# An attention stage ahead of two feed-forward blocks: squares summed by contiguous adds, the last score chunks split in halves, row sums divided out after the weight product, and six banks for that product

## The chip, the cores and the metric

The kernel runs on one core of one Trainium2 chip. The metric is the device time of one execution in microseconds; lower is better. The engines are named as in the profile: PE (TensorE), DVE (VectorE), ACT (ScalarE), POOL (GpSimd) and SP (SyncE, which issues the DMAs here).

## The reference

There are three parts in a row. The attention is over channels: q, k and v are 6016 x 256, and the attention matrix is only 256 x 256.

```
qn = q / (norm(q, axis=rows) + 1e-6)        # one norm per channel
kn = k / (norm(k, axis=rows) + 1e-6)
s  = kn.T @ qn / tau                        # 256 x 256, summed over the 6016 rows
a  = exp(s - max(s, -1));  a /= sum(a, -1) + 1e-9
x  = v @ a                                  # 6016 x 256
h  = x @ w_in1  (256 x 2048);  x = (h - tanh(h)) @ w_out1
h  = x @ w_in2  (256 x 2048);  out = where(h > 0, h, exp(min(h, 0)) - 1) @ w_out2
```

All data is float32. In the two blocks and in v's product, each float32 operand is split into a rounded high part and a low part (`_hi`, `_lo`), and three matmul passes replace one exact product.

## The kernel before

The kernel never forms x = v @ a. It multiplies the small matrices first: wf = a @ w_in1 (256 x 2048), and block 1 then computes v @ wf. So the work falls into an attention stage that ends in wf, and a main part of 12 tiles of 512 tokens (the last one shorter) in which PE runs four groups per step in a written order (A: v @ wf, B: w_out1, C: w_in2, D: w_out2). The change touches only the attention stage. Every engine has one instruction queue, written out by hand in program order; semaphores join them, and nothing is reordered at run time.

The 6016 rows are laid out as 47 rows per partition. They are loaded in chunks (`CHUNKS`, 1, 2, 2, 2 and then ten of 4 rows) into a ring of six buffers for k and six for q. For every chunk:

- SP issues the load of k and of q (L276). From the seventh chunk on it first waits until PE has multiplied the chunk that held the buffer (`chunk_multiplied`) and ACT has squared it (`squared`). After the chunks SP issues w_in1, the first tile of v (eight DMAs, L268), w_out1; after the scores w_in2; then the second tile of v; after the weight product w_out2.
- PE multiplies each row's k (as stationary operand, in two halves m = 0, 1 of 128 channels) with q, and adds all of it up in two banks, `scores_ps` (L352; the trace calls the banks `x_ps`). One such float32 matmul shows as two instructions in the trace.
- ACT squares k and q into `k_sq` and `q_sq` (L527), and may do so only when DVE has summed the chunk before (`summed`).
- DVE sums the squares over the rows with a reduction (L671). It reads the chunk's rows and the running sum, five rows of 256 for a full chunk, with the row as the innermost index, so at a stride of 256 elements, and writes one row of 256.

Then comes the end of the stage, in which little runs in parallel. When the last sum is there, PE adds it over the partitions by matmuls with a column of ones (L371), does the half m = 0 of the last chunk and one matmul of the other half of the last but one. ACT takes the root (L549), DVE corrects it by one Newton step, inverts, and puts 1/norm of q on a diagonal (L706 to L713); PE spreads that over the partitions with a matmul by ones (L385); ACT copies it to SBUF (L558). Meanwhile PE does the remaining halves m = 1. For m = 0 and then m = 1, DVE scales the scores (L719), takes the negated row maximum (L722), ACT forms exp and the row sum (L554), DVE adds 1e-9, inverts, and scales the row (L724 to L728), PE transposes it (L360), and ACT (m = 0) or DVE (m = 1) copies the result to `aT`. Last, PE forms wf in eight products of 128 x 512 (L403, four instructions each), in the order `WF_ORDER`, into four banks; ACT rounds each to wf_hi (L532) and DVE takes the difference wf_lo (L657). A product that takes a bank again waits for the split of the product before it in that bank. Between them DVE transposes the first tile of v (L687), and both engines split four pieces of w_out1.

The main part's first groups wait for the splits of the wf columns that they read.

Of the kernel before, what the change touches and what calls it, by code (L numbers as in the profile page):

```python
# [29 lines left out]
F32 = mybir.dt.float32  # L30
# [20 lines left out]
CHUNKS = [1, 2, 2, 2] + [4] * 10  # L51
# [3 lines left out]
SUM_ROW = CH + 1 if len(CHUNKS) % 2 else 0  # L55
assert sum(CHUNKS) == ROWS

# [22 lines left out]
WF_ORDER = [(0, 0), (1, 0), (0, 1), (1, 1), (2, 0), (2, 1), (3, 0), (3, 1)]  # L80
# [7 lines left out]
def attention_ffn_kernel(nc, q, k, v, tau, w_in1, w_out1, w_in2, w_out2, out):  # L88
    ctx = ExitStack()
    with ctx:  # L90
# [26 lines left out]
        row_sum = sb("row_sum", [P, CC])  # L117

        with ExitStack() as early:  # L120
            k_ring = [sb(f"k_ring{i}", [P, CH, C], stack=early) for i in range(RING)]
            q_ring = [sb(f"q_ring{i}", [P, CH, C], stack=early) for i in range(RING)]

            k_sq, q_sq = sb("k_sq", [P, CH + 2, C], stack=early), sb("q_sq", [P, CH + 2, C], stack=early)
            prob = sb("prob", [P, CC, C], stack=early)

            rq_diag, rq = sb("rq_diag", [P, CC, P], stack=early), sb("rq", [P, C], stack=early)
# [5 lines left out]
        with ExitStack() as early:  # L133
            stage_b = sb("stage_b", [P, CC * F], stack=early)
        x2_hi, x2_lo = sb("x2_hi", [P, CC, TILE], F32R), sb("x2_lo", [P, CC, TILE], F32R)
# [12 lines left out]
        scores_ps, aT_ps, wf_ps = x2_ps, h2_ps, (h2_ps, out_ps)  # L148
# [16 lines left out]
        sum_guarded, prob_ready, prob_transposed = sem("sum_guarded"), sem("prob_ready"), sem("prob_transposed")  # L165
# [175 lines left out]
        def _(pe):  # L341
# [15 lines left out]
            def transpose_prob(m):  # L357
                pe.wait_ge(prob_ready, m + 1)
                for d in range(CC):
                    last = nc.tensor.transpose(aT_ps[m][:, d * P:(d + 1) * P], prob[:, m, d * P:(d + 1) * P], ident[:, :])  # L360
                last.then_inc(prob_transposed, 1)

            for i in range(len(CHUNKS)):
                pe.wait_ge(loaded_k[i % RING], 16 * (i // RING + 1))
                pe.wait_ge(loaded_q[i % RING], 16 * (i // RING + 1))
                if i == len(CHUNKS) - 1:

                    pe.wait_ge(ones_ready, 1)
                    pe.wait_ge(summed, 2 * len(CHUNKS))
                    for col, (sq, m) in enumerate(((q_sq, 0), (q_sq, 1), (k_sq, 0), (k_sq, 1))):  # L370
                        last = nc.tensor.matmul(norms_ps[:, col:col + 1], sq[:, SUM_ROW, m * P:(m + 1) * P], ones[:, 0:1],  # L371
# [3 lines left out]
                if i < len(CHUNKS) - 2:  # L375
# [5 lines left out]
            scores(i - 1, 1, range(1))  # L381
            pe.wait_ge(rq_on_diagonal, CC)
            for m in range(CC):

                last = nc.tensor.matmul(rq_ps[:, m * P:(m + 1) * P], ones[:, :], rq_diag[:, m, :], start=m == 0, stop=True,  # L385
                                        skip_group_check=True)
            last.then_inc(rq_spread, 1)
# [9 lines left out]
            for n, (g, m) in enumerate(WF_ORDER):  # L397
                if g < 2:
                    pe.wait_ge(aT_ready[m], 1)
                else:  # L400
                    pe.wait_ge(wf_split, WF_ORDER.index((g - 2, m)) + 1)
                for d in range(CC):
                    last = nc.tensor.matmul(wf_ps[g % 2][m][:, :], aT[:, d, m * P:(m + 1) * P],  # L403
                                            w_in1_sb[:, d, g * 512:(g + 1) * 512], start=d == 0, stop=d == CC - 1)
# [113 lines left out]
        def _(act):  # L518
            act.wait_ge(ones_ready, 1)

            for i, rows in enumerate(CHUNKS):
                first = 1 if i % 2 == 0 else CH + 1 - rows
                for x, (ring, loaded, sq) in enumerate(((k_ring, loaded_k, k_sq), (q_ring, loaded_q, q_sq))):
# [23 lines left out]
            nc.scalar.activation(table_warm[:, 0:1], ones[:, 0:1], ACT.Sqrt)  # L547
# [8 lines left out]

            act.wait_ge(rq_spread, 1)
            nc.scalar.activation(rq[:, :], rq_ps[:, 0:C], ACT.Copy).then_inc(rq_ready, 1)  # L558
            exp_scores(0)
            act.wait_ge(prob_transposed, 1)  # L560
            nc.scalar.activation(aT[:, :, 0:P], aT_ps[0][:, 0:C].rearrange("p (d c) -> p d c", d=CC), ACT.Copy).then_inc(aT_ready[0], 1)
            exp_scores(1)
            round_wf(0)
# [90 lines left out]
        def _(dve):  # L654
# [4 lines left out]

            for i, rows in enumerate(CHUNKS):  # L660
                for x, sq in enumerate((k_sq, q_sq)):
                    if i == 0:
                        a, b, to = 1, 1 + rows, CH + 1
                    elif i % 2 == 0:
                        a, b, to = 0, 1 + rows, CH + 1
                    else:
                        a, b, to = CH + 1 - rows, CH + 2, 0
                    dve.wait_ge(squared, 2 * i + x + 1)
                    if i >= 1:
                        dve.wait_ge(summed, 2 * i + x - 1)  # L670
# [181 lines left out]
```

## Time and profile before

| | |
|---|---|
| median of 3 runs | 1117.67 us (1117.5 to 1117.76) |
| the profiled execution | 1117.52 us |
| its span | 1115.7 us |
| mean granted clock of PE | 0.992 |
| PE busy in the span | 1091.5 us, 98% |
| PE weight loads busy | 907.4 us, 81% |
| DVE busy | 728.2 us, 65% |
| ACT busy | 532.9 us, 48% |
| bytes read and written in HBM | 26.87 MB and 6.16 MB |

The span is the time from the first to the last instruction of the profiled execution; its own time is 1.8 us longer. A granted clock of 1.00 is 2.4 GHz, 0.50 is 1.2 GHz. Matmuls overlap one another, so the time that one is shown to take is longer than the distance between two starts. The averages hide the stages: the attention stage takes the first 83.5 us, and the main part the rest.

### The profile page before, as it was taken

How to read it: one execution, taken by the hardware profiler on the slowest of the kernel's cores; microseconds unless marked ns; L12 is line 12 of the kernel's file. 1: busy time of each engine (PE TensorE's matmuls, PEld its weight loads, DVE VectorE, ACT ScalarE, POOL GpSimd, SP SyncE). 2: the span in 40 equal slices, each digit the busy share in tenths (PEclk: the TensorE clock that was granted, in tenths of full speed). 3: DMA queues.
4: the chain of work that ended last, by engine and by line, in shares of the span. 5: the costliest groups of instructions: out<-in, count | busy, mean ns of one | idle time of the engine just before them, and what ended most of it. 6: DMA issues, size and time to landing. Idle time of an engine off the chain costs nothing.

```text
span 1115.7 us, 14119 instructions
## 1 busy us (share of the span) xinstructions
PE 1091.5 (98%) x4892; PEld 907.4 (81%) x4892; DVE 728.2 (65%) x1136; ACT 532.9 (48%) x889; POOL 0.8 (0%) x7
## 2 busy tenths in 40 slices
PE   8589999999999999999999999999999999999998
PEld 7458788888888888888888888888888888888898
DVE  7957766666666666666666576566665666666565
ACT  5446545544544544444444454454454454444443
POOL 0000000000000000000000000000000000000000
PEclk9889999999999999999999999999999999999999
DMA  9733001001011011011010010110110000000010
GB/s 351 261 95 88 7 1 20 10 10 19 1 20 19 1 19 19 0 19 19 0 19 12 7 19 0 19 19 0 19 19 0 14 13 6 0 3 17 1 20 15
DMA packets 105421, 33.42 MB, mean 30 GB/s; under 512 B 96816, under 2 KB 101552, under 8 KB 104880
## 3 DMA queue, kind: packets, MB, share of 16 engines
q1 hardware_dynamic: 105392, 33.04, 11.6%
q8 instruction: 17, 0.28, 0.1%
q14 instruction: 12, 0.10, 0.0%
HBM read 26.87 MB, written 6.16 MB: 30 GB/s over the span
## 4 chain that ended last, share of the span: by engine, by line
PE 93%; issue 4%; DVE 1%; ACT 1%; DMA 0%; SPq 0%; ACTq 0%; DVEq 0%
PE h_ps L344 15%; PE h_ps L346 15%; PE h_ps L345 15%; PE x_ps L344 8%; PE x_ps L345 8%; PE x_ps L346 8%; PE out_ps L344 8%; PE out_ps L345 8%; PE out_ps L346 8%; PE h_ps L403 1%; PE out_ps L403 1%; PE x_ps L352 0%; DVE q_sq L671 0%; DMA k_ring<-k_dram 0%; DVE g_lo L657 0%
## 5 line engine op out<-in xcount | busy, mean ns | idle before, releaser
L657 DVE TENSOR_TENSOR g_lo<-g,g_hi 128x512 fp32r<-128x512 f32 (+1 forms) x384 | 261.4, 681 | 225.1 <-ACT g_hi L598 116.6
L598 ACT ACTIVATE g_hi<-g 128x512 fp32r<-128x512 f32 (+1 forms) x192 | 119.5, 622 | 205.6 <-DVE g L766 205.2
L584 ACT ACTIVATE g_hi<-g 128x512 fp32r<-128x512 f32 (+1 forms) x192 | 119.7, 624 | 131.9 <-PE x_ps L346 70.4
L591 ACT ACTIVATE g<-h_ps 128x512 f32<-128x512 f32 (+1 forms) x192 | 113.1, 589 | 137.1 <-PE h_ps L346 136.2
L747 DVE TENSOR_TENSOR g<-h_ps,g 128x512 f32<-128x512 f32 (+1 forms) x192 | 129.6, 675 | 30.1 <-ACT g L577 29.9
L344 PE MATMUL h_ps<-vT_hi,wf_hi 128*128 128x512 f32 (+1 forms) x384 | 148.3, 386 | 0.0
L344 PE MATMUL x_ps<-g_hi,w_out_hi 128*128 128x512 f32 (+1 forms) x384 | 147.9, 385 | 0.2
L344 PE MATMUL h_ps<-x_hi,w_in_hi 128*128 128x512 f32 (+1 forms) x384 | 147.9, 385 | 0.1
L346 PE MATMUL h_ps<-x_hi,w_in_lo 128*128 128x512 f32 (+1 forms) x384 | 147.9, 385 | 0.0
L345 PE MATMUL h_ps<-x_lo,w_in_hi 128*128 128x512 f32 (+1 forms) x384 | 147.9, 385 | 0.0
L346 PE MATMUL h_ps<-vT_hi,wf_lo 128*128 128x512 f32 (+1 forms) x384 | 147.9, 385 | 0.0
L762 DVE TENSOR_SCALAR g<-g 128x512 f32<-128x512 f32 (+1 forms) x192 | 81.0, 422 | 102.3 <-ACT g L591 101.8
L345 PE MATMUL h_ps<-vT_lo,wf_hi 128*128 128x512 f32 (+1 forms) x384 | 147.8, 385 | 0.0
L345 PE MATMUL x_ps<-g_lo,w_out_hi 128*128 128x512 f32 (+1 forms) x384 | 147.7, 385 | 0.0
L346 PE MATMUL x_ps<-g_hi,w_out_lo 128*128 128x512 f32 (+1 forms) x384 | 147.7, 385 | 0.0
L577 ACT ACTIVATE g<-h_ps 128x512 f32<-128x512 f32 (+1 forms) x192 | 112.8, 587 | 54.3 <-PE h_ps L346 54.3
L346 PE MATMUL out_ps<-g_hi,w_out_lo 128*128 128x512 f32 x352 | 137.2, 390 | 0.0
L345 PE MATMUL out_ps<-g_lo,w_out_hi 128*128 128x512 f32 x352 | 137.1, 390 | 0.0
L344 PE MATMUL out_ps<-g_hi,w_out_hi 128*128 128x512 f32 x352 | 137.1, 389 | 0.0
L766 DVE TENSOR_TENSOR g<-h_ps,g 128x512 f32<-128x512 f32 (+1 forms) x192 | 130.6, 680 | 6.1
L344 PEld LDWEIGHTS x_ps<-g_hi,w_out_hi 128*128 128x128 f32 x384 | 72.1, 188 | 15.0 <-DVE g_lo L657 1.2
L344 PEld LDWEIGHTS h_ps<-vT_hi,wf_hi 128*128 128x128 f32 x384 | 72.1, 188 | 15.0 <-DVE g L747 0.5
(85 smaller groups left out, 1112.9 us busy)
## 6 DMA issues: line engine op xcount, KB each, us to landing
v_blocks<-v_dram SPq DMA_DIRECT2D x88, 64.0 KB, 2.2
out_dram<-out_sb SPq DMA_DIRECT2D x88, 64.0 KB, 1.8
k_ring<-k_dram SPq DMA_DIRECT2D x10, 512.0 KB, 8.4
q_ring<-q_dram SPq DMA_DIRECT2D x10, 512.0 KB, 9.3
stage_a<-moe_w_in_dram SPq DMA_DIRECT2D x1, 2048.0 KB, 13.0
stage_b<-moe_w_out_dram SPq DMA_DIRECT2D x1, 2048.0 KB, 8.5
w_in_raw<-moe_w_in_dram SPq DMA_DIRECT2D x1, 2048.0 KB, 9.4
stage_a<-moe_w_out_dram SPq DMA_DIRECT2D x1, 2048.0 KB, 8.4
```

The lines of the kernel that those rows point to most:

```text
L344: nc.tensor.matmul(ps, w_hi, m_hi, start=start, stop=False, **kw)
L345: nc.tensor.matmul(ps, w_hi, m_lo, start=False, stop=False, **kw)
L346: return nc.tensor.matmul(ps, w_lo, m_hi, start=False, stop=stop, **kw)
L403: last = nc.tensor.matmul(wf_ps[g % 2][m][:, :], aT[:, d, m * P:(m + 1) * P], w_in1_sb[:, d, g * 512:(g + 1) * 512], start=d == 0, stop=d ...
L577: nc.scalar.activation(g1[i % 2][:, 0:n], h1_ps[i % 2][:, 0:n], ACT.Tanh).then_inc(tanh_ready, 1)
L584: nc.scalar.activation(g1_hi[i % 2][:, 0:n], g1[i % 2][:, 0:n], ACT.Copy).then_inc(g1_rounded, 1)
L591: nc.scalar.activation(g2[i % 2][:, 0:n], h2_ps[i % 2][:, 0:n], ACT.Exp).then_inc(exp2_ready, 1)
L598: nc.scalar.activation(g2_hi[i % 2][:, 0:n], g2[i % 2][:, 0:n], ACT.Copy).then_inc(g2_rounded, 1)
L657: return nc.vector.tensor_tensor(lo, x, hi.bitcast(F32), ALU.subtract)
L747: nc.vector.tensor_tensor(g1[i % 2][:, 0:n], h1_ps[i % 2][:, 0:n], g1[i % 2][:, 0:n], ALU.subtract).then_inc(g1_ready, 1)
L762: nc.vector.tensor_scalar(g2[i % 2][:, 0:n], g2[i % 2][:, 0:n], 1.0, -1.0, ALU.min, ALU.add).then_inc(elu_low, 1)
L766: nc.vector.tensor_tensor(g2[i % 2][:, 0:n], h2_ps[i % 2][:, 0:n], g2[i % 2][:, 0:n], ALU.max).then_inc(g2_ready, 1)
```

## The change

What it does, in words:

- `CHUNKS` becomes 1, 1, 2, 3, nine of 4, 2, 2 (15 chunks instead of 14).
- The squares of the first three chunks (four rows) are written straight into four rows of `k_acc` and `q_acc`. Each later chunk's squares go to `k_sq` / `q_sq`, and DVE adds them row by row to the running rows with a two-operand add over contiguous memory. Before the last chunk the four running rows are folded to two, and after it to one.
- PE leaves out the half m = 1 of the last four chunks (12 rows, was six) until after the norms. The spread of 1/norm stands after the first of them.
- The row sum is no longer divided out of `prob`. PE transposes the exp itself; 1/sum goes to `inv_sum`, and is applied per partition where wf is rounded and split.
- The transposes of m = 0 come after all scores; those of m = 1 after the first product. ACT makes both copies to `aT`. `WF_ORDER` does the four column groups of m = 0 first, and the eight products use six banks, of which two are used twice.
- DVE transposes v's first tile before the first two splits. ACT loads the table of Sqrt before the squares. `prob`, `rq_diag` and `rq` lie at other addresses.

```diff
-CHUNKS = [1, 2, 2, 2] + [4] * 10
+CHUNKS = [1, 1, 2, 3] + [4] * 9 + [2, 2]
...
-SUM_ROW = CH + 1 if len(CHUNKS) % 2 else 0
+DIRECT = 3
+TAIL = 4
+LAST = len(CHUNKS) - 1
...
-WF_ORDER = [(0, 0), (1, 0), (0, 1), (1, 1), (2, 0), (2, 1), (3, 0), (3, 1)]
+WF_ORDER = [(0, 0), (1, 0), (2, 0), (3, 0), (0, 1), (1, 1), (2, 1), (3, 1)]
+def summed_through(i, x):
+    return 2 * (i - DIRECT) + x + 1 + (2 if i == LAST else 0)
+SUMMED_FOLD = [summed_through(LAST - 1, 1) + x + 1 for x in range(2)]
+SUMMED_ALL = summed_through(LAST, 1) + 2
...
-        scores_ps, aT_ps, wf_ps = x2_ps, h2_ps, (h2_ps, out_ps)
+        scores_ps, aT_ps = x2_ps, h2_ps
+        wf_ps = out_ps + x2_ps + out_ps + h2_ps
...
# PE
             def transpose_prob(m):
-                pe.wait_ge(prob_ready, m + 1)
+                pe.wait_ge(exp_ready, m + 1)
...
-                if i == len(CHUNKS) - 1:
+                if i == LAST:
                     pe.wait_ge(ones_ready, 1)
-                    pe.wait_ge(summed, 2 * len(CHUNKS))
+                    pe.wait_ge(summed, SUMMED_ALL)
...
                 last = scores(i, 0, range(CHUNKS[i]))
-                if i < len(CHUNKS) - 2:
+                if i <= LAST - TAIL:
                     scores(i, 1, range(CHUNKS[i])).then_inc(chunk_multiplied, 1)
             last.then_inc(scores_ready, 1)
-            scores(i - 1, 1, range(1))
-            pe.wait_ge(rq_on_diagonal, CC)
...
-            scores(i - 1, 1, range(1, CHUNKS[i - 1]))
-            scores(i, 1, range(CHUNKS[i] - 1))
+            for i in range(LAST - TAIL + 1, LAST + 1):
+                if i == LAST - TAIL + 2:
+                    pe.wait_ge(rq_on_diagonal, CC)
...
+                last = scores(i, 1, range(CHUNKS[i]))
+            last.then_inc(scores_ready, 1)
             transpose_prob(0)
-            scores(i, 1, [CHUNKS[i] - 1]).then_inc(scores_ready, 1)
...
             for n, (g, m) in enumerate(WF_ORDER):
-                if g < 2:
-                    pe.wait_ge(aT_ready[m], 1)
-                else:
-                    pe.wait_ge(wf_split, WF_ORDER.index((g - 2, m)) + 1)
+                pe.wait_ge(aT_ready[m], 1)
+                if n in (4, 5):
+                    pe.wait_ge(wf_split, n - 3)
...
-                    if n == 1 and d == 0:
-                        transpose_prob(1)
                 last.then_inc(wf_multiplied, 1)
+                if n == 0:
+                    transpose_prob(1)
...
# ACT
             act.wait_ge(ones_ready, 1)
+            nc.scalar.activation(table_warm[:, 0:1], ones[:, 0:1], ACT.Sqrt)
...
-                    if i >= 1:
-                        act.wait_ge(summed, 2 * (i - 1) + x + 1)
-                    nc.scalar.activation(sq[:, first:first + rows, :], ring[i % RING][:, 0:rows, :], ACT.Square).then_inc(squared, 1)
+                    if i > DIRECT:
+                        act.wait_ge(summed, summed_through(i - 1, x))
+                    to = acc[:, ROW0[i]:ROW0[i] + rows, :] if i < DIRECT else sq[:, 0:rows, :]
+                    nc.scalar.activation(to, ring[i % RING][:, 0:rows, :], ACT.Square).then_inc(squared, 1)
...
-                nc.scalar.activation(wf_hi[:, m, g * 512:(g + 1) * 512], wf_ps[g % 2][m][:, :], ACT.Copy).then_inc(wf_rounded, 1)
+                act.wait_ge(sum_inverted, m + 1)
+                nc.scalar.activation(wf_hi[:, m, g * 512:(g + 1) * 512], wf_ps[n][:, :], ACT.Copy,
+                                     scale=inv_sum[:, m:m + 1]).then_inc(wf_rounded, 1)
...
             exp_scores(0)
+            copy_aT(0)
             exp_scores(1)
+            copy_aT(1)
             round_wf(0)
             round_wf(1)
...
# DVE
+            def add_rows(x, to, a, b):
+                acc = (k_acc, q_acc)[x]
+                return nc.vector.tensor_tensor(acc[:, 0:to, :], a, b, ALU.add)
+
             for i, rows in enumerate(CHUNKS):
...
+                if i == LAST:
+                    for x, acc in enumerate((k_acc, q_acc)):
+                        dve.wait_ge(summed, summed_through(i - 1, x))
+                        add_rows(x, 2, acc[:, 0:2, :], acc[:, 2:4, :]).then_inc(summed, 1)
+                for x, (sq, acc) in enumerate(((k_sq, k_acc), (q_sq, q_acc))):
+                    if i < DIRECT:
+                        continue
                     dve.wait_ge(squared, 2 * i + x + 1)
...
-                    nc.vector.tensor_reduce(sq[:, to, :], sq[:, a:b, :].rearrange("p r c -> p c r"), AX.X, ALU.add).then_inc(summed, 1)
+                    add_rows(x, rows, acc[:, 0:rows, :], sq[:, 0:rows, :]).then_inc(summed, 1)
+            for x, acc in enumerate((k_acc, q_acc)):
+                dve.wait_ge(summed, summed_through(LAST, x))
+                add_rows(x, 1, acc[:, 0:1, :], acc[:, 1:2, :]).then_inc(summed, 1)
...
-                minus(wf_lo[:, m, cols], wf_ps[g % 2][m][:, :], wf_hi[:, m, cols]).then_inc(wf_split, 1)
+                nc.vector.scalar_tensor_tensor(out=wf_lo[:, m, cols], in0=wf_ps[n][:, :], scalar=inv_sum[:, m:m + 1],
+                                               in1=wf_hi[:, m, cols].bitcast(F32), op0=ALU.mult,
+                                               op1=ALU.subtract).then_inc(wf_split, 1)
...
+            for m in range(CC):
                 dve.wait_ge(exp_ready, m + 1)
                 nc.vector.tensor_scalar_add(row_sum[:, m:m + 1], row_sum[:, m:m + 1], 1e-9).then_inc(sum_guarded, 1)
                 dve.wait_ge(sum_guarded, m + 1)
-                nc.vector.reciprocal(row_sum[:, m:m + 1], row_sum[:, m:m + 1]).then_inc(sum_inverted, 1)
-                dve.wait_ge(sum_inverted, m + 1)
-                nc.vector.tensor_scalar(prob[:, m, :], prob[:, m, :], row_sum[:, m:m + 1], None, ALU.mult).then_inc(prob_ready, 1)
-            dve.wait_ge(prob_transposed, 2)
-            nc.vector.tensor_copy(aT[:, :, P:2 * P], aT_ps[1][:, 0:C].rearrange("p (d c) -> p d c", d=CC)).then_inc(aT_ready[1], 1)
+                nc.vector.reciprocal(inv_sum[:, m:m + 1], row_sum[:, m:m + 1]).then_inc(sum_inverted, 1)
+            for cc in range(CC):
+                transpose_v(0, cc)
             split_wf(0)
             split_wf(1)
-            for cc in range(CC):
-                transpose_v(0, cc)
```

## Rows read from the trace of the kernel before

**Rows 1.** Stretches: us, length, PE PEld DVE ACT POOL busy, clock, DMA share, GB/s.

```profile
43.34:58.42 15.08, 0.00 (x1) 0.03 (x1) 15.00 (x8) 7.15 (x8) 0.00 (x0) 0.66 0.49 149
58.42:65.24 6.82, 6.82 (x22) 5.92 (x23) 1.64 (x9) 1.66 (x3) 0.00 (x0) 0.51 0.00 1
...
69.33:83.52 14.19, 14.19 (x35) 6.47 (x36) 10.53 (x20) 7.34 (x14) 0.00 (x0) 1.00 0.63 186
83.52:1115.70 1032.18, 1028.17 (x4657) 859.51 (x4655) 662.18 (x1074) 494.21 (x837) 0.00 (x0) 1.00 0.07 13
```

**Rows 2.** Chain of waits, 55 to 69 us: start us, us, what.

```profile
55.95 2.34 DVE q_sq L671
...
58.42 1.84 PE out_ps L371 x8
60.26 4.47 PE x_ps L352 x10
64.73 0.68 PE out_ps L385 x4
...
65.44 0.39 ACT rq L558
...
66.90 0.61 ACT prob L554 x2
...
67.92 0.36 DVE prob L728
...
68.33 0.44 PE h_ps L360 x2
```

**Rows 3.** DVE: groups by line and shape before 84 us, then three timeline rows.

```profile
L671 DVE TENSOR_REDUCE k_sq<-k_sq 128x256 f32<-128x1280 f32 x10 | 23.8, 2381 | 0.2 <-ACT k_sq L527 0.2
...
L657 DVE TENSOR_TENSOR w_out_lo<-stage_b,w_out_hi 128x512 fp32r<-128x512 f32 x3 | 2.0, 681 | 0.0
...
61.81 0.48 DVE L713 TENSOR_SCALAR rq_diag<-ident,inv_norm 128x128 f32<-128x128 f32 x2
...
77.11 0.69 DVE L657 TENSOR_TENSOR wf_lo<-h_ps,wf_hi 128x512 fp32r<-128x512 f32 x1
77.71 0.68 DVE L657 TENSOR_TENSOR wf_lo<-out_ps,wf_hi 128x512 fp32r<-128x512 f32 x1
```

**Rows 4.** ACT: groups by line and shape before 84 us.

```profile
L527 ACT ACTIVATE k_sq<-k_ring 128x1024 f32<-128x1024 f32 x10 | 10.6, 1058 | 11.7 <-DVE k_sq L671 11.7
...
L527 ACT ACT_TABLE_LOAD x1 | 1.3, 1283 | 2.9 <-DMA k_ring<-k_dram 2.9
...
L554 ACT ACTIVATE prob<-prob,neg_max 128x256 f32<-128x256 f32 x2 | 1.0, 508 | 2.1 <-DVE neg_max L722 2.1
```

**Rows 5.** PE timeline, then L352 before 12 us and from 20 to 30 us.

```profile
3.51 2.05 PE L352 MATMUL x_ps<-q_ring,k_ring 128*128 128x256 f32 x4 [3.51 <-DMA q_ring<-q_dram]
6.71 36.63 PE L352 MATMUL x_ps<-q_ring,k_ring 128*128 128x256 f32 x160 [1.15 <-DMA q_ring<-q_dram]
...
L352 PE MATMUL x_ps<-q_ring,k_ring x20: 379/634/767, 3.5 to 11.9; 128*128 128x256 f32 x20
...
L352 PE MATMUL x_ps<-q_ring,k_ring x48: 379/379/379, 19.6 to 29.8; 128*128 128x256 f32 x48
```

**Rows 6.** DMA issues on SP's queue, timeline.

```profile
10.49 0.33 SPq L276 DMA_DIRECT2D k_ring<-k_dram  x1
...
12.29 0.33 SPq L276 DMA_DIRECT2D k_ring<-k_dram  x1
...
29.47 13.76 SPq L268 DMA_DIRECT2D v_blocks<-v_dram  x8
```

**Rows 7.** Stretches with DMA: clock, DMA share and GB/s are the last three.

```profile
0.00:4.50 4.50, 1.00 0.40 85
4.50:5.20 0.70, 1.00 0.71 243
...
13.00:30.00 17.00, 17.00 (x80) 14.97 (x79) 17.00 (x8) 7.91 (x8) 0.00 (x0) 1.00 1.03 410
```

More of the change, by code:

```diff
@@ L54 @@
 RING = 6
-SUM_ROW = CH + 1 if len(CHUNKS) % 2 else 0
-assert sum(CHUNKS) == ROWS
+DIRECT = 3
+TAIL = 4
+LAST = len(CHUNKS) - 1
+assert sum(CHUNKS) == ROWS and sum(CHUNKS[:DIRECT]) == CH and CHUNKS[LAST] == 2
 BLOCK = 32
@@ L116, in attention_ffn_kernel @@
         neg_max = sb("neg_max", [P, CC])
-        row_sum = sb("row_sum", [P, CC])
+        row_sum, inv_sum = sb("row_sum", [P, CC]), sb("inv_sum", [P, CC])
         with ExitStack() as early:
@@ L365, in _ @@
                 pe.wait_ge(loaded_q[i % RING], 16 * (i // RING + 1))
[L366 removed]
+                if i == LAST:
                     pe.wait_ge(ones_ready, 1)
[L369 to L371 removed]
+                    pe.wait_ge(summed, SUMMED_ALL)
+                    for col, (acc, m) in enumerate(((q_acc, 0), (q_acc, 1), (k_acc, 0), (k_acc, 1))):
+                        last = nc.tensor.matmul(norms_ps[:, col:col + 1], acc[:, 0, m * P:(m + 1) * P], ones[:, 0:1],
                                                 start=col == 0, stop=True, skip_group_check=True)
@@ L374, in _ @@
                 last = scores(i, 0, range(CHUNKS[i]))
-                if i < len(CHUNKS) - 2:
+                if i <= LAST - TAIL:
                     scores(i, 1, range(CHUNKS[i])).then_inc(chunk_multiplied, 1)
             last.then_inc(scores_ready, 1)
-            scores(i - 1, 1, range(1))
-            pe.wait_ge(rq_on_diagonal, CC)
[L383 to L387, printed above, removed]
-            scores(i - 1, 1, range(1, CHUNKS[i - 1]))
-            scores(i, 1, range(CHUNKS[i] - 1))
+            for i in range(LAST - TAIL + 1, LAST + 1):
+                if i == LAST - TAIL + 2:
+                    pe.wait_ge(rq_on_diagonal, CC)
+                    for m in range(CC):
+                        last = nc.tensor.matmul(rq_ps[:, m * P:(m + 1) * P], ones[:, :], rq_diag[:, m, :], start=m == 0, stop=True,
+                                                skip_group_check=True)
+                    last.then_inc(rq_spread, 1)
+                last = scores(i, 1, range(CHUNKS[i]))
+            last.then_inc(scores_ready, 1)
             transpose_prob(0)
-            scores(i, 1, [CHUNKS[i] - 1]).then_inc(scores_ready, 1)
             w_in1_sb = stage_a[:, :].rearrange("p (a f) -> p a f", a=CC)
@@ L519, in _ @@
             act.wait_ge(ones_ready, 1)
+            nc.scalar.activation(table_warm[:, 0:1], ones[:, 0:1], ACT.Sqrt)
             for i, rows in enumerate(CHUNKS):
-                first = 1 if i % 2 == 0 else CH + 1 - rows
-                for x, (ring, loaded, sq) in enumerate(((k_ring, loaded_k, k_sq), (q_ring, loaded_q, q_sq))):
+                for x, (ring, loaded, sq, acc) in enumerate(((k_ring, loaded_k, k_sq, k_acc), (q_ring, loaded_q, q_sq, q_acc))):
                     act.wait_ge(loaded[i % RING], 16 * (i // RING + 1))
-                    if i >= 1:
-                        act.wait_ge(summed, 2 * (i - 1) + x + 1)
-                    nc.scalar.activation(sq[:, first:first + rows, :], ring[i % RING][:, 0:rows, :], ACT.Square).then_inc(squared, 1)
+                    if i > DIRECT:
+                        act.wait_ge(summed, summed_through(i - 1, x))
+                    to = acc[:, ROW0[i]:ROW0[i] + rows, :] if i < DIRECT else sq[:, 0:rows, :]
+                    nc.scalar.activation(to, ring[i % RING][:, 0:rows, :], ACT.Square).then_inc(squared, 1)
             def round_wf(n):
@@ L722, in _ @@
                 nc.vector.tensor_reduce(neg_max[:, m:m + 1], prob[:, m, :], AX.X, ALU.max, negate=True).then_inc(max_ready, 1)
+            for m in range(CC):
                 dve.wait_ge(exp_ready, m + 1)
```

31 lines of the change are left out of this document (14 added, 17 removed).

## The prediction

> **What bounds the kernel now.** I read the table of stages first, then the chain of waits, then DVE, ACT, PE and the DMA issues of the first 84 us. In the table [rows 1] the reader is to see that from 83.52 us on PE is busy 1028 of 1032 us: that part is untouched and full, so all that this change can move lies before it. In there, PE is idle from 43.34 to 58.42 us while DVE is busy 15.00 of 15.08 us, and then works 6.82 us at a granted clock of 0.51. The chain [rows 2] says the same by instruction: it runs through the reductions of L671 up to 58.28, then over the norms (L371), ten score matmuls, the spread of 1/norm (L385), one trip through ACT and DVE, the transposes and the 32 weight-product matmuls, which end at 83.52. The twenty 128x1280 reductions take 2.38 us each [rows 3] and leave ACT waiting 11.7 us for DVE ahead of k's squares alone [rows 4]. So the stage is paced by DVE at 4.6 us per chunk of four rows, while PE needs 16 x 0.215 = 3.45 us (next paragraph).
>
> **PE's price list.** A float32 score matmul is two instructions. At full clock 48 of them start between 19.6 and 29.8 us, about 0.215 us each. The ten at 60.26 took 4.47 us, 0.447 each, at the half clock [rows 2, 5]. At the start they also ran at half speed: the median of the first 20 is 634 ns long, against 379 later [rows 5], although the clock column there shows 1.00. The ring's slots say when that ended, since SP issues the next load when a chunk is through: chunk 1 (8 instructions from 6.71) was done just before 10.49, 0.46 each; chunk 2 before 12.29, 0.225 each [rows 5, 6].
>
> **Part 1: contiguous adds.** Gone are 20 reductions of 2.38 us and the small ones. New on DVE are 18 adds of 128x1024, two of 768, six of 512 and two of 256. No add of this size stands in the trace. The nearest row is a two-operand float32 operation on 128x512 of SBUF, 681 ns long; two of that shape that read PSUM start 0.60 us apart [rows 3]. Below, the cost of the 1024 can't be under that 0.60; above, the 1280 reduction gives 2.38. I take twice the start distance, 1.20, because the operand is contiguous like that row's. Sum: 18x1.20 + 2x0.90 + 6x0.60 + 2x0.35 = 27.7 us. The first needed chunk (rows 4 to 6) lands by about 9.7, and its squares take 0.8, so DVE could be done at 10.5 + 27.7 = 38.2. The hand-over is a little slower: ACT may square chunk i+1 of k only after DVE added chunk i, so one turn is 1.06 (square) + 0.03 + 1.29 (add with its tail) + 0.10 = 2.48 us, and nine of them put the last sum near 39.5 to 40. DMA brings four rows of k and q (1.05 MB) in 2.55 us at the 410 GB/s of [rows 7], the same pace. Both are under PE's 3.45, so PE becomes the pacer. By the starts alone DVE stays hidden up to (41.3 - 10.5 - 6.1)/18 = 1.37 us per add.
>
> The Trainium skill (VectorE: DVE Perf Modes, Mode 2×_2P) says that a float32 tensor_tensor stays at one element per cycle, since both read ports carry operands; 512 more elements at its 0.96 GHz would be an estimated 0.53 us on top of 681 ns. That is 1.21 us against the 1.29 I use for one add's length, and no row here shows the size.
>
> **Part 2: when PE reaches the norms.** It must do 80 row-halves first, as before (there 42 + 38, now 45 + 35): 160 instructions. It starts at 3.51 again. Chunk 0 ended at 5.56 and then PE waited 1.15 us for the 256 KB transfers of chunk 1 [rows 5]. The new chunk 1 is 128 KB each, and lands at about 5.2, since 0.55 MB have arrived by then (4.5 x 85 GB/s and 0.7 x 243) [rows 7], so that gap goes. With the clock rising at 10.4 as before, (10.4 - 3.5)/0.447 = 15 instructions are done by then and the other 145 take 31.2: 41.6. If it rises earlier because the matmuls now follow one another, by as much as the 3.7 us from 6.7 to 10.4, that gives 1.8, less about 1.0 that the arrivals of chunks 2 and 3 take back: 40.8. I take 41.3. So the norms start 17.1 us earlier.
>
> Ring slots: chunks 11 to 14 keep their second half and their buffers, and nothing is loaded after them. Chunk 14 is issued when chunk 8 is through (rows up to 27, about 30.5) and lands near 34.5. Behind it on SP's queue stand w_in1, v and w_out1. v's eight issues lasted 13.8 us to 43.28 [rows 6], held by the backlog and not by their number; now they end near 45, w_in1 has landed near 40 (14.4 MB at 410 GB/s take 35 us; needed at about 50), v near 46 (needed at 51.3), w_out1, 2.1 MB behind them at that rate or a little less, near 52 (needed at 58). All hidden, with 5 us or more.
>
> **Part 3: the half clock.** PE no longer idles before the norms, so I price that stretch at full clock. Before: norms 1.84, ten matmuls 4.47, spread 0.68, twelve matmuls and the wait up to the transposes 2.91, then 1.00 to the first weight product and 14.19 to 83.52: 25.1 [rows 1, 2]. After: norms 1.84/2 = 0.9; 12 matmuls (chunk 14 first half, chunk 11 second) 2.6; spread 0.45; 16 matmuls 3.45; transposes and aT copy 1.0; products 14.2. Sum 22.6, so 2.5 us less. The diagonal is ready 2.03 us after the norms (60.26 to 61.81 + 0.48 [rows 2, 3]), under the 2.6 of cover: no wait, 0.5 us to spare. In those rows PE had idled 15 us; then the clock was 0.51 from 58.42 to 65.24, and 1.00 from 69.33 on [rows 1].
>
> The Trainium skill (TensorE: Matmul & The Clock Gate, Part 1) says that the throttled state is the default and activity releases it. By that rule the stretch runs at 2.4 GHz if nothing else stalls PE. The trace agrees with the two levels, 0.51 and 1.00 [rows 1].
>
> **Part 4: softmax with the sum divided out later.** Transposes now wait for exp alone; the guard, the reciprocal and the 0.36 us scaling leave the path, 67.51 to 68.28, 0.77 us [rows 2]. But the chain from spread to exp (65.42 to 66.90 + 0.61, 2.1 us [rows 2]) has 3.45 us of matmuls over it, so this is worth nothing beyond the 0.3 us wait already in the sum. Second half: scores end, then 0.5 + 0.45 + 0.6 and hand-overs give exp 1.8 us later; PE meets its transposes after 1.0 + 1.7 = 2.7. Hidden. What comes instead is a per-partition scale in eight ACT copies and eight DVE subtractions, 0.6 to 0.7 us each now. The exp with its per-partition bias took 508 ns for 256 columns [rows 4], the plain copy of rq 0.39 us [rows 2], so I take 0 to 0.12 us more each. A product then costs ACT 0.72 and a w_out1 piece 0.6, 1.3 us against PE's 1.72 per product, and DVE the same (681 ns a piece [rows 3]). Hidden. Nothing is gained either, as PE does not wait for them.
>
> **Part 5: six banks.** Products 5 and 6 reuse banks, and wait for splits 1 and 2. These are ready some 4 us after the first product ends; PE comes 5.2 us after. Before, with four banks, the 32 instructions took 14.19 us, 0.43 each and 0.2 for the transposes among them [rows 1], so no wait was left to win. So 0. The order by column group makes the first main group wait for split 5 instead of 3; product 5 has ended 5.2 us before that, and its rounding and split take 1.4. The last splits and w_out1 pieces stand at the same distance from the end. The Sqrt table is loaded before the squares, 1.28 us beside the first transfer: 0. Moved buffers: no time.
>
> **Sum.** 17.1 + 2.5 = 19.6 us off the profiled execution's 1117.52 (span 1115.7 and 1.8 around it): 1097.9. The median shown is 0.15 higher: **1098.0**. Its own range is 1096.6 to 1099.5.
>
> **Rivals.**
> - DVE stays last, 0.13. For: adds longer than 1.37 us, or hand-overs of 2.6, put the last sum behind 41.3; the margin is one to two us. Each 0.1 us per add costs 1.8 us and an idle PE may fall to half clock, 2.5 more. At 1.5 us: 1098.0 + 2.3 + up to 2.5 = 1100 to 1103. At the reduction's 2.38: about 1115. Against: the 681 ns row.
> - Tail partly at half clock, 0.06. If PE idles or the clock falls for another reason in the 28 matmuls, each costs 0.23 more: 6 us, 1104. Against: 1.00 from 13 to 30 us [rows 7], with PE as steadily fed as it is to be here.
> - Loads late, 0.05. v transposes now stand ahead of splits 1 and 2 on DVE; v later than 54.5 us would hold product 5 one for one: 1100 to 1103.
> - Square forces a table switch, 0.03. L527 loaded its own table before [rows 4]. A load of 1.28 on the root would pass the 0.5 us spare: 1098.8. The Trainium skill (ScalarE: Activation LUTs, Table sets) says that cheap functions are filler of every set; no row here shows it for this pair.
> - Slower, 0.02. The DVE adds cost by what they read and write. The 1280 reduction is 1.86 ns per element read; an add reads 2048: 3.8 us. From 2.5 us on it is worse than now, at 3.8 the norms start near 85: 1143. The 681 ns for 1024 elements read speaks against it.
>
> Forecast 0.71. The 8-in-10 range is 1096.3 to 1101.5: the forecast, table and small versions of the DVE and load cases. Faster by over 0.2% (2.2 us, what can be told from no change) 0.97, same 0.01, slower 0.02.
>
> **What would show it.** After: adds of 1.2 to 1.3 us at 128x1024; no idle of PE before the norms at 41.3 and a granted clock near 1.00 from there to the products; first product at 49.5 to 50; main part starting at 63.9. A norms matmul waiting for DVE refutes part 1, a clock near 0.5 after it part 3, a wait at the fifth product part 5. A main part other than 1032 us refutes the base of it all.

## The result, and the profile after

The change makes the kernel faster by less than half of what was forecast: 1108.84 us median (1108.33 to 1109.34, 4 runs) against 1117.67, a ratio of 0.9924 (95% interval 0.991 to 0.9938). The forecast was 1098.0, its range 1096.3 to 1101.5. The profiled execution took 1108.33 us, its span is 1106.5.

First the table of stages of the changed kernel (stretch, length, busy time of PE, PEld, DVE, ACT, POOL, granted clock, DMA share, GB/s). The cuts are the start of the norms, of the first weight product, and of the main part.

```profile
0.00:42.11 42.11, 37.83 (x163) 32.22 (x163) 28.41 (x29) 27.55 (x32) 0.84 (x7) 1.00 0.95 349
42.11:50.28 8.17, 7.61 (x43) 6.62 (x42) 3.25 (x13) 3.03 (x7) 0.00 (x0) 1.00 0.89 247
50.28:64.47 14.19, 14.19 (x35) 6.49 (x36) 9.70 (x19) 8.27 (x15) 0.00 (x0) 1.00 0.71 212
...
64.47:1106.50 1042.03, 1037.97 (x4657) 859.46 (x4655) 662.25 (x1074) 494.45 (x837) 0.00 (x0) 1.00 0.07 13
```

Against [rows 1] the idle stretch is gone, the clock is 1.00 through the tail, and the main part begins at 64.47 instead of 83.52: 19.05 us gained. But the main part takes 1042.03 us instead of 1032.18, with the same 4657 matmuls, the same clock of 1.00 and no more idle time of PE (4.06 against 4.01): 9.85 us are given back. 19.05 - 9.85 = 9.2 is the whole difference of the two profiled executions.

The chain of waits up to the main part (start us, us, what), where [rows 2] had the reductions:

```profile
10.79 31.32 PE x_ps L364 x144
42.11 0.79 PE out_ps L383 x8
42.90 2.70 PE x_ps L364 x12
45.60 0.44 PE out_ps L398 x4
46.04 3.46 PE x_ps L364 x16
49.50 0.23 PE h_ps L372 x2
49.75 0.40 ACT aT L572
50.28 1.95 PE out_ps L414 x4
...
61.04 3.43 PE h_ps L414 x8
```

It is PE all the way, but for one copy by ACT. The timeline of DVE, for [rows 3]: adds of 1024 elements per partition take 1.23 us and start 1.28 apart, and the last sum ends 1.5 us before the norms.

```profile
13.01 1.22 DVE L681 TENSOR_TENSOR k_acc<-k_acc,k_sq 128x1024 f32<-128x1024 f32 x1 [0.49 <-ACT k_sq L539]
14.29 1.23 DVE L681 TENSOR_TENSOR q_acc<-q_acc,q_sq 128x1024 f32<-128x1024 f32 x1
...
40.19 0.42 DVE L681 TENSOR_TENSOR q_acc<-q_acc 128x256 f32<-128x256 f32 x1
```

PE's timeline at the start, for [rows 5]: the first gap is gone (sixteen instructions in one piece from 3.92), 0.36 us is left at 10.4. The distances between starts fall from 0.427 to 0.216 us at 9.4 us, so the clock was full from there; before, they did so at 10.5.

```profile
3.92 6.51 PE L364 MATMUL x_ps<-q_ring,k_ring 128*128 128x256 f32 x16 [3.92 <-DMA q_ring<-q_dram]
10.79 31.32 PE L364 MATMUL x_ps<-q_ring,k_ring 128*128 128x256 f32 x144 [0.36 <-DMA q_ring<-q_dram]
```

So where do 9.85 us go? The groups of matmuls of the main part by line and shape (count, busy us, mean ns of one):

```profile
L356 PE MATMUL h_ps<-vT_hi,wf_hi 128*128 128x512 f32 x352 | 138.8, 394 | 0.0
L357 PE MATMUL h_ps<-vT_lo,wf_hi 128*128 128x512 f32 x352 | 138.8, 394 | 0.0
L356 PE MATMUL h_ps<-x_hi,w_in_hi 128*128 128x512 f32 x352 | 138.6, 394 | 0.0
```

### The profile page after: what moved, and what is told of

The parts are those of the page before. It is cut to its first block, busy times and chain, and to the rows that moved or that the text cites. A ratio compares the mean times of both kernels' runs of the same rounds, so it can differ in the third digit from the quotient of the medians.

```text
span 1106.5 us, 14123 instructions
## 1 busy us (share of the span) xinstructions
PE 1097.6 (99%) x4892; PEld 904.8 (82%) x4892; DVE 703.6 (64%) x1133; ACT 533.3 (48%) x891; POOL 0.8 (0%) x7
## 4 chain that ended last, share of the span: by engine, by line
PE 98%; DVE 1%; DMA 1%; ACT 0%; SPq 0%; issue 0%; ACTq 0%
PE h_ps L356 16%; PE h_ps L358 15%; PE h_ps L357 15%; PE x_ps L358 8%; PE x_ps L356 8%; PE out_ps L358 8%; PE out_ps L356 8%; PE x_ps L357 8%; PE out_ps L357 8%; PE x_ps L364 3%; PE out_ps L414 1%; DMA q_ring<-q_dram 1%; PE h_ps L414 0%; PE x_ps L414 0%; DVE g_lo L675 0%; SPq L288 0%
## 5 line engine op out<-in xcount | busy, mean ns | idle before, releaser
L357 PEld LDWEIGHTS h_ps<-vT_lo,wf_hi 128*128 128x128 f32 x384 | 72.1, 188 | 16.1 <-issue 0.2
```

Source lines behind the costliest of these rows:

```text
L357: nc.tensor.matmul(ps, w_hi, m_lo, start=False, stop=False, **kw)
```

## The experiments

Twelve of sixteen vary addresses; "shift" is always in bytes per partition and against the kernel before. The table first. The third column is the time for one step of 24 matmuls in tiles 1 and later (the second iteration and on), from their start times in the trace; the last is how many matmuls are seen in the 200 us from 500 to 700. The kernel before, run beside them, was at 1117.2 to 1117.8 each time; the last four have one run each.

| kernel | what is shifted | ns per step | matmuls | us, median |
|---|---|---|---|---|
| before | | 5440 | 884 | 1117.67 |
| changed | block 2 by 32 | 5506 | 873 | 1108.84 |
| e2_odd_before | before, block 2 by 32 | 5506 | 873 | 1126.96 |
| e1_even_after | changed, block 2 by 64 | 5494 | 874 | 1107.76 |
| e3_all_odd | changed, block 1 by 32, block 2 by 96 | 5494 | 875 | 1107.17 |
| e4_even_128 | changed, block 2 by 128 | 5460 | 880 | 1102.49 |
| f2_plus_256 | changed, block 2 by 256 | 5440 | 884 | 1099.60 |
| f1_same_addresses | changed, no shift | 5440 | 884 | 1098.32 |
| f9_moving_32_off | f1, block 2 by 256, and block 1's streamed operands 32 off | 5560 | 865 | 1118.61 |
| g1_moving_128_off | streamed 128 off the weights, both blocks | 5600 | 859 | 1123.02 |
| i_moving_64_off | the same, 64 off | 5493, from 290 us on 5600 | 859 | 1118.90 |
| i_moving_192_off | the same, 192 off | 5600 | 859 | 1125.25 |
| i_moving_224_off | the same, 224 off | 5600 | 859 | 1125.54 |
| i_others_32_off | only tensors PE does not read, by 32 | 5440 | 884 | 1098.79 |

**Is it addresses at all?** The kernel before with an unused tensor, and the changed one with a wider `inv_sum`:

```diff
 # e2_odd_before
         row_sum = sb("row_sum", [P, CC])
+        pad = sb("pad", [P, 8])
 # e1_even_after; e4_even_128 the same with [P, 32]
-        row_sum, inv_sum = sb("row_sum", [P, CC]), sb("inv_sum", [P, CC])
+        row_sum, inv_sum = sb("row_sum", [P, CC]), sb("inv_sum", [P, 16])
 # e3_all_odd: as e1, and
+        pad = sb("pad", [P, 8])
         wf_hi, wf_lo = sb("wf_hi", [P, CC, F], F32R), sb("wf_lo", [P, CC, F], F32R)
```

> The kernel before, with one unused tensor of 32 bytes per partition after row_sum; instructions stay. The tensors of block 2 start 32 bytes past a multiple of 64. Address theory: 1117.7 + 9.8 = 1127.5 us, the steps of 24 matmuls from tile 1 on at 5.50 us instead of 5.44. Rival: 1117.7.

> The changed kernel with inv_sum allocated as 128x16 instead of 128x2 (64 bytes per partition instead of the 32 that a tensor takes at least); instructions and order stay. All tensors allocated after it (w_out2, w_in2, x2, g2, out_sb) then start at a multiple of 64 bytes again, as in the kernel before. Address theory: the main part of 1042.0 us goes back to 1032.2, so the execution takes 1108.3 - 9.8 = 1098.5 us. Rival (the main part is slower through its place in the instruction memory, or through what the attention stage leaves behind): nothing of that changes, 1108 to 1109.

> The changed kernel, inv_sum 64 bytes wide, and one unused tensor of 32 bytes in front of everything, so that all tensors, those of block 1 and of the attention stage too, start 32 bytes past a multiple of 64. Address theory: block 2 costs 9.8 us as in the changed kernel, and block 1 and the attention stage about the same again: 1098.5 + 9.8 + 10 to 11 = 1118 to 1120 us; if only mixing tensors of both kinds costs, 1098.5. Rival: 1108 to 1109.

> The changed kernel with inv_sum 128 bytes wide: later tensors start at a multiple of 128 bytes, where with 64 bytes they start at an odd multiple of 64. Address theory with 64 as the step: 1098.5, the same as with inv_sum 64 wide. If 128 is the step, this one alone is at 1098.5 and the other between. Rival: 1108 to 1109.

e2 took 1126.96 us (ratio 1.0083, interval 1.0069 to 1.0096), 9.3 above its base. Its main part:

```profile
83.18:1125.10 1041.92, 1037.88 (x4657) 859.54 (x4655) 662.31 (x1074) 493.98 (x837) 0.00 (x0) 1.00 0.07 13
```

This is the kernel before with no instruction changed, and its main part is as slow as that of the changed one, 1041.92 to 1042.03. So addresses alone do it. But e1 refutes my first form of it, that starting at a multiple of 64 is what counts: 1107.76, hardly better. e3 has the same step as e1 to the nanosecond although everything lies 32 bytes further (its 1107.17 us refute the 1118 to 1120 of that form too), so it is the distance between tensors that counts and not the place of any. e4's 128 bytes cost a third of what 32 do.

**Is it all of the 9.85 us, and does it repeat?** f1 puts `inv_sum` where later tensors lie over it; f2 makes it 256 bytes wide.

```diff
 # f1_same_addresses
-        row_sum, inv_sum = sb("row_sum", [P, CC]), sb("inv_sum", [P, CC])
+        row_sum = sb("row_sum", [P, CC])
...
             rq_diag, rq = sb("rq_diag", [P, CC, P], stack=early), sb("rq", [P, C], stack=early)
+            inv_sum = sb("inv_sum", [P, CC], stack=early)
```

> The changed kernel with inv_sum allocated behind rq, in a part that x2 to out_sb take over later, so that w_out2, w_in2, x2, g2 and out_sb lie at exactly the addresses they have in the kernel before. So far: 32, 64 and 128 bytes of shift of block 2's tensors against block 1's cost 66, 54 and 20 ns per step of 24 matmuls, and moving everything by another 32 changed nothing. Distance theory (what counts is the distance between the tensors of the two blocks, and the old distance was a good one): no extra, the main part at 1032.2 us and the execution at 1098.3 to 1098.8. Rival (the order or the place of the new instructions costs a part of the 9.8 us as well): above 1100.

> The changed kernel with inv_sum 256 bytes wide: block 2's tensors move by 256 bytes against the kernel before. If the cost repeats with 256 bytes, as 66, 54, 20 ns at 32, 64, 128 suggest, or ends there: 1098.5. If it goes on falling slowly or repeats only with 512 or more: 1099 to 1103. Theory without distance: 1108.

f1: 1098.32 us (1097.71 to 1099.17, 5 runs), ratio 0.9832 (0.9819 to 0.9845). Its main part is back at the old length:

```profile
64.21:1096.50 1032.29, 1028.18 (x4657) 859.50 (x4655) 662.40 (x1074) 494.73 (x837) 0.00 (x0) 1.00 0.07 13
500.00:700.00 200.00, 200.00 (x884) 165.47 (x883) 126.45 (x201) 93.63 (x156) 0.00 (x0) 1.00 0.08 13
```

It is the fastest kernel of this study, faster than both, and it holds every line of the change but the place of an 8-byte tensor. f2 has the same main part (5440 ns per step); its profiled execution reached the norms 2 us later than f1's (43.66 against 41.69). PE waited 1.18 us there for the third chunk's transfers, against 0.42, and its matmuls went on starting 0.427 us apart up to 13.1 us, against 9.0 in f1.

**Distance between what?** Either PE's weight load against its streamed operand, or PE against DVE and ACT.

```diff
 # f9_moving_32_off, on f1
+        pad_a = sb("pad_a", [P, 8])
         v_blocks = sb("v_blocks", [P, CC, TILE])
...
         row_sum = sb("row_sum", [P, CC])
+        pad_b = sb("pad_b", [P, 56])
 # g1_moving_128_off, on f1: pads of 32 elements ahead of v_blocks, after row_sum
 # and ahead of x2_hi; i_moving_d_off: d/4, (256 - d)/4 and d/4 elements
 # i_others_32_off, on f1: 8 elements ahead of v_blocks, g1, g2 and out_sb,
 # and 56 ahead of vT_hi, g1_hi and g2_hi
```

> The changed kernel with a shift of 256 bytes for block 2 (as in f2), and 32 unused bytes ahead of v_blocks, so that block 1's moving operands (vT, g1) lie 32 bytes off against its weights (wf, w_out1), while block 2's own operands keep their distance. If what counts is the distance between the weights being loaded and the operand being streamed, also within a block, the groups A and B leave 226.7 ns per matmul in the middle of a group too, and the first iteration (block 1 alone) is slower than 5.44 us per 24: 1102 to 1112 us. If only the change from one block to the other costs: as f2, at most 66 ns per step more.

> f1 with unused tensors such that in both blocks the streamed operands (vT, g1, x2, g2) start 128 bytes off, modulo 256, against the weights (wf, w_out1, w_in2, w_out2); the weights of both blocks agree modulo 256. 32 off in block 1 alone cost 4 to 7 ns per matmul. If the distance weights to streamed operand sets the time of every matmul: another constant than 226.7 ns, on either side of it (each ns is 4.6 us in all; 128 off cost the least of the distances between blocks, so up to 3 ns more, 1098 to 1112; below 1098 if 0 is not the best distance). If only unequal distances cost, 1098.3.

> As g1, with the streamed operands of both blocks 64 bytes off against their weights (modulo 256) instead of 128. If the cost is one of collisions between the two reads of PE, that repeat with 256 bytes: a constant per matmul other than 226.7 ns, between 226 and 234; between blocks 64 off cost more than 128 off, within a block the order may differ. Total 1098 + 4.6 us per ns. If it is a matter of DVE or ACT: no fixed pattern per matmul.

> As g1, 192 bytes off, which is -64 modulo 256. If the collision depends only on how far the two reads are apart, the same as 64 off. If it matters which one is ahead, another value, and one of the two could be below 226.7 ns, the first sign of a faster layout: under 1098 us.

> As g1, 224 bytes off, which is -32 modulo 256. Block 1 at +32 took 230 to 236 ns per matmul. Same reasoning: the same for a symmetric collision (233 ns, 1128 us), another value if the order counts.

> f1 with only those tensors moved by 32 bytes that PE never reads in the main part (v_blocks, vT, g1, g2, out_sb); everything that PE reads keeps its old place modulo 256. If the two reads of PE collide with each other: 226.7 ns per matmul everywhere, 1098 to 1100 us. If PE's reads collide with those of DVE and ACT: more than 226.7, up to the 9.8 us of the changed kernel, 1100 to 1108.

The stretch from 500 to 700 us of g1, then of i_others_32_off:

```profile
500.00:700.00 200.00, 200.00 (x859) 160.89 (x858) 123.68 (x197) 91.19 (x151) 0.00 (x0) 1.00 0.08 13
```

```profile
500.00:700.00 200.00, 200.00 (x884) 165.56 (x883) 126.83 (x202) 93.48 (x155) 0.00 (x0) 1.00 0.08 13
```

Moving every tensor that PE does not read in the main part changes nothing (1098.79, one run). Moving the streamed operands against the weights costs up to 160 ns per step, 25 us in all (g1), at a clock of 1.00 and with PE always busy. f9 and g1 lie above the 1112 us that I gave either at most. In f9's first iteration, block 1 alone with its operands 32 off, 24 matmuls take 5600 ns, against 5440 in f2. The simplest reading is that the two reads of PE, the next weights and the streamed operand, hinder each other. It is argued in part: i_others_32_off leaves the tensors that ACT and DVE write and PE reads where they were, so the writes to them were not tested against the weight loads. The pattern speaks against such writes: it repeats every two or three matmuls, to within a nanosecond, while ACT and DVE do other work from one matmul to the next. The mean distances between starts of the 24 matmuls of one step, group by group (A: v @ wf, B: w_out1, C: w_in2, D: w_out2), show it in the order of time, in ns (i_64 once up to 285 us and once from 290 us on):

```
before    A 227 227 227 227 227 227  B 227 227 227 227 227 227  C 227 227 227 227 227 227  D 227 227 227 227 227 227
changed   A 230 236 229 232 231 227  B 227 227 227 227 227 235  C 230 224 231 236 228 233  D 231 227 227 227 227 235
g1        A 238 229 237 229 238 229  B 238 229 237 229 238 229  C 238 229 237 229 238 229  D 238 229 237 229 238 229
i_64 <285 A 226 229 232 226 229 232  B 226 229 232 226 229 232  C 226 229 232 226 229 232  D 226 229 232 226 229 232
i_64 >290 A 233 233 233 233 233 233  B 233 233 233 233 233 233  C 233 233 233 233 233 233  D 233 233 233 233 233 233
```

In the changed kernel weights and streamed operand agree modulo 256 within each block, but the blocks lie 32 bytes apart. The disturbance begins with the last matmul of B, while the first weights of C are being loaded, and again with the last of D, and is gone after the seven (C) or five (A) that follow. Where the two operands disagree within a block (g1, i_64), the whole step is slow. 192 and 224 off cost as much as 128. No distance that was tried beats 0.

i_64 shows that the addresses do not settle it alone. Up to 285 us every step in the order A, B, C, D takes 5493 ns, and from 290 us on every one takes 5600, in one execution and at the same addresses. Two stretches of equal length, one on each side:

```profile
115.00:280.00 165.00, 165.00 (x722) 135.39 (x721) 106.99 (x170) 80.57 (x134) 0.00 (x0) 1.00 0.06 10
300.00:465.00 165.00, 165.00 (x709) 133.66 (x708) 101.75 (x162) 76.19 (x126) 0.00 (x0) 1.00 0.06 10
```

So 64 off ends at the same 233.3 ns per matmul as 128, 192 and 224, and its lower total of 1118.90 us comes from the early steps. The change falls into iteration 3, the first that runs in a loop (`FIRST_LOOPED`), while iterations 1 and 2 are written out. Whether the loop is the reason, no run shows; no other kernel of the table changes its pace there.

**The parts of the change, on f1.** Strided adds (`"p r c -> p c r"` on all three operands of each add), the halves (`TAIL = 2`), and the two parts that were priced at nothing.

```diff
 # f7_strided_adds
-                return nc.vector.tensor_tensor(acc[:, 0:to, :], a, b, ALU.add)
+                swap = lambda x: x.rearrange("p r c -> p c r")
+                return nc.vector.tensor_tensor(swap(acc[:, 0:to, :]), swap(a), swap(b), ALU.add)
 # h1_tail_2; h3_adds_alone is this and h2
-TAIL = 4
+TAIL = 2
 # h2_scaled_four_banks: prob scaled by DVE before the transposes, and
-WF_ORDER = [(0, 0), (1, 0), (2, 0), (3, 0), (0, 1), (1, 1), (2, 1), (3, 1)]
+WF_ORDER = [(0, 0), (1, 0), (0, 1), (1, 1), (2, 0), (2, 1), (3, 0), (3, 1)]
...
-        wf_ps = out_ps + x2_ps + out_ps + h2_ps
+        wf_ps = [(h2_ps, out_ps)[g % 2][m] for g, m in WF_ORDER]
...
-                act.wait_ge(sum_inverted, m + 1)
...
+                nc.vector.tensor_scalar(prob[:, m, :], prob[:, m, :], inv_sum[:, m:m + 1], None, ALU.mult).then_inc(prob_ready, 1)
```

> f1 (block 2 at the addresses of before) with the adds of part 1 walked in the old order, row innermost, so that each operand is read at a stride of 256 elements; same number of adds and elements. If the stride was what made the reductions slow (1.86 ns per element at 1280), an add of 1024 takes up to 1.9 us instead of 1.23, DVE needs some 40 us for all, PE waits for the norms until about 51 and falls to half clock: 1106 to 1112 us. If the reduction as an operation was slow, not the stride: 1.23 us per add and 1098.5.

1116.09 us (1114.71 to 1118.63, 10 runs), ratio 0.9988 (0.9978 to 0.9997). An add of 1024 took 2.55 us in the old order of walking, not the 1.9 at most that I gave it:

```profile
L683 DVE TENSOR_TENSOR q_acc<-q_acc,q_sq 128x1024 f32<-128x1024 f32 x9 | 23.1, 2563 | 0.0
L683 DVE TENSOR_TENSOR k_acc<-k_acc,k_sq 128x1024 f32<-128x1024 f32 x9 | 23.0, 2550 | 0.0
```

```profile
57.34 0.98 PE L384 MATMUL out_ps<-ones,q_acc 128*128 128x1 f32 x4 [14.70 <-DVE q_acc L683]
```

PE waits 14.70 us again, and nearly all of the gain is gone. The same add over the same elements takes 2.55 us in the one order and 1.23 in the other, and that alone undoes the gain. That the order also made the old reductions slow (2.38 us for 1280 elements read) is likely and not shown: f7 walks the output in that order too, and no run has a reduction in another order.

> f1 (the change with block 2's tensors at the old addresses, 1098.3) with TAIL = 2: only the last two chunks' second halves stand after the norms, the spread between them. The matmuls are the same in number. By the prediction's part 3: cover of the norm steps falls from 12 matmuls (2.6 us) to 8 (1.72) against 2.03 and hand-overs, a wait of 0.4; after the spread 4 matmuls (0.86) stand over the 2.1 us up to exp, a wait of 1.2. Sum 1.6 to 1.7 us: 1099.9 to 1100.0. Rival (the earlier end of the sums or the full clock is all that counts, not the order): 1098.3.

> f1 with parts 4 and 5 undone: the row sum is divided out of prob before the transposes, plain rounding and splitting of wf, the old order of the products in four banks. By the prediction both are hidden: 0.77 us more in the chain of 2.1 lies under 3.45 us of matmuls, the second half's exp comes at about the time of its transposes, and products 5 to 8 find their splits done: 1098.3, up to 1098.6. Rival (one of them is what keeps PE fed): 1099.5 or more, with a wait at L373 or L415.

> f1 with parts 4 and 5 undone and TAIL = 2: what is left of the change is contiguous adds, the chunk sizes and the table load. The sums are in time, the clock stays at 1.00. Waits: 0.4 before the spread, and (2.1 + 0.77) - 0.86 = 2.0 before the first transposes. 1098.3 + 2.4 = 1100.7, so the adds alone bring 17 of 19.3 us. Rival (the gain needs the halves too): 1104 or more.

h2: 1099.54 us (1097.97 to 1099.74), ratio 0.9839 (0.9825 to 0.9852), not told apart from f1's. From the norms to the main part both take 21.96 us (41.69 to 63.65 in f1, 42.38 to 64.34 in h2), so the scaling after the product, the order and the six banks are worth nothing here, as forecast. (The copies to `aT` by ACT and the early transposes of v stay in h2.)

h1: 1101.22 us (1100.12 to 1101.33), ratio 0.9854 (0.9839 to 0.9869). The two waits are where they were put, 0.25 and 1.28 us (PE's timeline):

```profile
49.08 0.71 PE L399 MATMUL out_ps<-rq_diag,ones 128*128 128x128 f32 x4 [0.25 <-DVE rq_diag L744]
...
51.94 0.44 PE L373 MATMUL h_ps<-ident,prob 128*128 128x128 f32 x2 [1.28 <-ACT prob L568]
```

With what drains around them the tail is 2.0 us longer (1.6 to 1.7 expected); the other 0.9 us of its profiled execution lie in the first transfers, ahead of the norms.

h3: 1102.44 us (1101.07 to 1105.37, 4 runs), ratio 0.9864 (0.9848 to 0.9879). What is left in it of the change, the adds with the chunk sizes and the early table load, brings 15 of f1's 19 us (17 expected). The spread is wide for a reason that its profiled execution shows (PE's timeline, then stretches):

```profile
53.19 0.54 PE L373 MATMUL h_ps<-ident,prob 128*128 128x128 f32 x2 [2.06 <-DVE prob L755]
54.30 3.75 PE L415 MATMUL h_ps<-stage_a,aT 128*128 128x512 f32 x4 [0.57 <-ACT aT L571]
```

```profile
51.20:53.19 1.99, 0.00 (x1) 0.00 (x1) 1.22 (x6) 0.60 (x2) 0.00 (x0) 1.00 1.16 387
53.19:54.30 1.11, 0.54 (x3) 0.23 (x3) 0.76 (x2) 0.53 (x2) 0.00 (x0) 0.59 0.99 375
53.19:60.96 7.77, 7.20 (x12) 3.21 (x13) 3.33 (x8) 1.74 (x5) 0.00 (x0) 0.56 0.88 298
```

After waits of 0.25 and 2.06 us, and ahead of that of 0.57, the clock fell to its lower level, 1.2 GHz, for most of 7.8 us, and the first product took 3.75 instead of 1.96. The four runs are at mean clocks of 1.000, 1.000, 0.998 and 0.997 with 1101.1, 1101.3, 1103.6 and 1105.4 us: with the same code it falls in some executions and not in others. So the halves and the shorter chain are worth more than their waits: with either of them (h2, h1) all runs stayed at 0.999 or 1.000. By the Trainium skill (TensorE: Matmul & The Clock Gate, Part 1) activity releases the throttle. This trace agrees: after 7 us in which PE was nearly always busy the clock is 1.00 again, from 60.96 to 70 us.

## Why the prediction was wrong

The step that failed is the first sentence of it: that from 83.52 us on the work is "untouched and full", so that "all that this change can move lies before it", and with it "Moved buffers: no time" in part 5. The first is true of the instructions and of PE's busy share, and both are beside the point. The main part's matmuls were busy before and after; on average each starts 2.7 ns later after the one ahead, 9.85 us in all. I had read the diff's new buffers for who waits for them, and not for where they push the others. The text did name what would show it ("a main part other than 1032 us refutes the base of it all"), but gave no rival to it and no part of the range, and that, not only the middle, made the range too narrow. A case "the main part does not stay as it is", over 4600 matmuls where 1 ns each is 4.6 us, deserved a chance that a diff with a new and three moved allocations plainly gives it.

Everything else came out, and f1 at 1098.32 is what the sum of 1098.0 describes. By its steps:

- Part 1, right. Adds of 1.23 us (1.20 taken by the start distance, 1.29 by the length; measured 1.28 and 1.23). A chunk's turn was 2.56 us, not 2.48, and the two adds back to back fill it, not the hand-over. Last sum at 40.6 (39.5 to 40), PE not waiting. The cushion was 1.5 us.
- Part 2, right in kind, 0.8 us late: norms at 42.11, not 41.3. The gap before chunk 1 went, and the clock rose at 9.4, a microsecond earlier than the 10.4 that the sum took over from before. But PE began 0.4 us later than before, at 3.92, and waited 0.36 us for chunk 3's q. That 41.3 came this near is partly luck: the moment of the rise differs between executions of the same instructions (9.0 us in f1, 13.1 in f2), and with it the norms (41.69 and 43.66).
- Part 3, right: 22.36 us from the norms to the main part (22.6), clock 1.00, the diagonal in time. 25.1 to 22.36 is 2.7 us (2.5 forecast).
- Part 4, right: h2 shows nothing in it. The scaled copies took 0.69 us against 0.60, the splits 0.75 against 0.69.
- Part 5, right for the banks: product 5 starts with no wait. Wrong for the buffers.
- Of the rivals, "tail partly at half clock" did not hold for the change, but h3 shows it is real, after waits of 0.25 and 2.06 us. "DVE stays last" holds for f7.

What stays open is how PE's reads collide. The runs show that the distance between weights and streamed operand decides whether there is a cost, and that 0 is the best of 0, 64, 128, 192 and 224 (and 32 in block 1); that the cost repeats with 256 bytes rests on one run between blocks, f2. They do not show why a disturbance between blocks is gone after five to seven matmuls, nor why i_64 changes its pace between 285 and 290 us.

## What to carry to other kernels

A new tensor is a change to every tensor allocated behind it: before pricing a diff, list whose address moves, and put small new ones at the end or where others lie over them. In a part where one engine is busy all the time, look at the distance between starts, along the whole part, and not at busy shares or waits, and give "that part does not stay the same" a chance of its own. Reduce over rows by adding whole rows, in the order in which they lie in memory.

## What the runs showed of the hardware that was not expected

- A float32r matmul of 128x512, back to back with others, starts 226.7 ns after the last when its weights and its streamed operand agree modulo 256 bytes in the partition; 229 and 238 in turn (233.3 in the mean) at 128 off, the same mean at 192 and 224, and at 32 in f9's first iteration. The clock column stays at 1.00 and the engine at 100% busy.
- At 64 off the matmuls of one execution ran at two paces with the same addresses: 228.9 ns per matmul up to 285 us, 233.3 from 290 us on.
- The distance also counts from one matmul to the next: 32 bytes between the operands of two blocks whose groups alternate cost 66 ns per 24 matmuls, 64 bytes 54, 128 bytes 20, 256 bytes none.
- A two-operand add of 128x1024 float32 takes 1.23 us over contiguous memory and 2.55 with the innermost step at 256 elements.
- PE's clock fell after idle times of 0.25 and 2.06 us one soon after the other (h3, profiled execution; mean clocks 0.997 and 0.998 in two of its four, 1.000 in the others); waits of 0.25, 1.28 and 0.56 us (h1) left it at 1.00 in the profiled one.
